# First head of an attention kernel: its loads on three queues, its split in pieces, TensorE turning the identity meanwhile

## The reference

```python
scores = scale * np.matmul(q, k.transpose(0, 1, 3, 2))
thresh = np.max(scores, axis=-1, keepdims=True) - tau
scores = np.where(scores >= thresh, scores, -1000000000.0)
scores = scores - np.max(scores, axis=-1, keepdims=True)
attn = np.exp(scores)
attn = attn / (np.sum(attn, axis=-1, keepdims=True) + 1e-09)
x = np.matmul(attn, v)            # then (tokens, heads * width)
g = gate(x @ w_in);  x = g @ w_out    # twice, with two gates
```

## Time and profile before

| | us |
|---|---|
| median of three runs | 1115.55 (1115.53 to 1116.26) |
| the profiled execution, its own time | 1116.74 |
| its span in the trace | 1115.0 |
| TensorE busy | 1098.8 |
| first matmul starts | 7.68 |

### The profile page before, as it was taken

The page is one execution under the profiler, slowest core; times in us unless marked ns, Lnnn a source line. Parts: engine busy times, 40 slices in busy tenths (PEclk is TensorE's granted clock), DMA queues, the critical chain, the costliest instruction groups (busy, mean ns, idle before and its releaser), DMA issues.

```text
span 1115.0 us, 15233 instructions
## 1 busy us (share of the span) xinstructions
PE 1098.8 (99%) x6064; PEld 880.3 (79%) x6064; DVE 423.6 (38%) x903; ACT 489.9 (44%) x882; POOL 263.5 (24%) x179
## 2 busy tenths in 40 slices
PE   6999999999999999999999999999999999999998
PEld 5767676767668888889988888888888888888897
DVE  6878887878831211112121112123223223222222
ACT  5778787877743332223232234442233233232232
POOL 6686558556621300000000015430000000000000
PEclk9999999999999999999999999999999999999999
DMA  7432223223022000000000022300010010010010
GB/s 221 132 108 65 77 74 97 65 66 96 11 76 76 1 1 1 1 1 1 1 1 1 19 75 96 96 18 1 1 38 1 1 38 0 1 39 1 1 39 20
DMA packets 42488, 46.09 MB, mean 41 GB/s; under 512 B 3504, under 2 KB 30128, under 8 KB 42416
## 3 DMA queue, kind: packets, MB, share of 16 engines
q1 hardware_dynamic: 42416, 45.10, 13.6%
HBM read 40.37 MB, written 4.72 MB: 40 GB/s over the span
## 4 chain that ended last, share of the span: by engine, by line
PE 97%; DVE 1%; ACT 1%; issue 1%; DMA 0%; SPq 0%; DVEq 0%
PE banks L489 35%; PE banks L462 12%; PE banks L464 12%; PE banks L463 12%; PE banks L409 8%; PE banks L356 7%; PE banks L368 5%; PE banks L364 3%; PE banks L389 2%; DVE probs L709 0%; DVE neg_max L725 0%; ACT exps L572 0%; DMA q_raw<-qT 0%; ACT probsT L537 0%; DVE totals L741 0%
## 5 line engine op out<-in xcount | busy, mean ns | idle before, releaser
L770 DVE SCALAR_TENSOR_TENSOR g_low<-gate,g_high 128x512 fp32r<-128x512 f32 (+1 forms) x160 | 102.7, 642 | 473.2 <-ACT g_high L645 473.2
L462 PE MATMUL banks<-x_low,w_in_high 128*128 128x512 f32 (+1 forms) x640 | 235.9, 369 | 0.0
L463 PE MATMUL banks<-x_high,w_in_low 128*128 128x512 f32 (+1 forms) x640 | 235.5, 368 | 0.0
L464 PE MATMUL banks<-x_high,w_in_high 128*128 128x512 f32 (+1 forms) x640 | 235.5, 368 | 0.0
L645 ACT ACTIVATE g_high<-gate 128x512 fp32r<-128x512 f32 (+1 forms) x160 | 94.3, 589 | 309.6 <-PE banks L489 309.1
L462 PEld LDWEIGHTS banks<-x_low,w_in_high 128*128 128x128 f32 x640 | 120.6, 188 | 21.2 <-issue 0.6
L463 PEld LDWEIGHTS banks<-x_high,w_in_low 128*128 128x128 f32 x640 | 120.6, 188 | 20.5
L464 PEld LDWEIGHTS banks<-x_high,w_in_high 128*128 128x128 f32 x640 | 120.7, 189 | 20.0
L725 DVE TENSOR_REDUCE neg_max<-banks 128x1 f32<-128x576 f32 x144 | 108.7, 755 | 50.3 <-PE banks L356 50.1
L489 PE MATMUL banks<-g_low,w_out_high 128*128 128x512 f32 (+1 forms) x320 | 118.0, 369 | 0.8 <-issue 0.8
L489 PE MATMUL banks<-g_high,w_out_low 128*128 128x512 f32 (+1 forms) x320 | 117.8, 368 | 0.0
(11 more groups left out here) (59 smaller groups left out, 1430.1 us busy)
## 6 DMA issues: line engine op xcount, KB each, us to landing
q_raw<-qT SPq DMA_DIRECT2D x64, 144.0 KB, 2.8
k_raw<-kT SPq DMA_DIRECT2D x64, 144.0 KB, 2.8
w_in_raw<-w_in SPq DMA_DIRECT2D x16, 512.0 KB, 4.3
w_out_raw<-w_out SPq DMA_DIRECT2D x16, 512.0 KB, 4.7
out<-x SPq DMA_DIRECT2D x18, 256.0 KB, 2.9
values<-v SPq DMA_DIRECT2D x16, 256.0 KB, 3.1
values<-v SPq DMA_DIRECT2D x16, 32.0 KB, 2.8
tau_in<-tau SPq DMA_DIRECT2D x1, 0.5 KB, 2.8
```

The source lines that it names most:

```text
L462: nc.tensor.matmul(bank, w_in_high[:, t, cols], low, start=(t == 0), stop=False)
L463: nc.tensor.matmul(bank, w_in_low[:, t, cols], high, start=False, stop=False)
L464: mm = nc.tensor.matmul(bank, w_in_high[:, t, cols], high, start=False, stop=(t == KT - 1))
L770: nc.vector.scalar_tensor_tensor(out=g_low[:, f % 2, 0:width], in0=gate[:, f % 2, 0:width], scalar=1 / 6 if layer_of(c) else 1.0, in1=f32( ...
```

## The change

1. **Queues.** k of head 0 is issued by ScalarE as its first two instructions, ahead of its table load; tau is issued by GpSimd ahead of the clearing of `ident`; SP starts with q of head 0.
2. **Split of head 0 in pieces.** ScalarE rounds k in two halves of 288 columns. VectorE's order becomes: q's first 128 columns (scale and round; scale and remainder in one instruction), k's remainder in two halves, and last q's other 448 columns. The in-place scaling of L696 is gone, so the semaphore `q_scaled[0]` gets one increment less, and `split_head` waits for it accordingly. Tile 0 waits for the first q piece and, half by half, for the two k pieces; tile 1 waits for the rest of q.
3. **Turning the identity.** Ahead of tile 0 TensorE does 14 transposes of `ident` against itself into a bank that nobody reads.

```diff
+    WARM = 14
@@ sync
-            sp.dma_start(tau_in[:, :], tau.partition_broadcast(P)).then_inc(tau_loaded, 16)
...
+                if (it, k) == (0, 0):
+
+                    return
                 after(sp, k_low_ready[(k - 2) % HEADS_IT], it + k // 2)
@@ tensor, score_tile
-                if i in (0, MAIN):
+                if t == 0:
+                    pe.wait_ge(first_q_low, 1)
+                if t == 1:
+                    pe.wait_ge(q_low_ready[0], 1)
+                if t > 0 and i in (0, MAIN):
...
+                    if t == 0:
+                        pe.wait_ge((first_k_low, k_low_ready[0])[half], 1)
...
+            for j in range(WARM):
+                nc.tensor.transpose(turned[:, 0:P], ident[:, :], ident[:, :])
@@ scalar
+            for half in range(2):
+                act.dma_start(k_raw[0][DH * half:DH * half + DH, :],
+                              kT[bass.ds(0, 1)].rearrange("a d n -> (a d) n")).then_inc(k_loaded[0], 16)
...
-            round_k(0, 0)
+            act.wait_ge(k_loaded[0], 32)
+            for half in range(2):
+                cols = slice(HALF * half, HALF * half + HALF)
+                nc.scalar.copy(k_high[0][:, cols], k_raw[0][:, cols]).then_inc((first_k_high, k_high_ready[0])[half], 1)
@@ vector
-            q_place = q_stack[0][:, 0:SEQ]
-            nc.vector.tensor_scalar(q_place, q_raw[0][:, :], q_scale[:, :], None, ALU.mult).then_inc(q_high_ready[0], 1)
...
+            def split_first_q(cols, rounded, count):
+
+                place, low = q_stack[0][:, cols], slice(DH, P)
+                nc.vector.tensor_scalar(place, q_raw[0][:, cols], q_scale[:, :], None, ALU.mult).then_inc(rounded, 1)
+                dve.wait_ge(rounded, count)
+                return nc.vector.scalar_tensor_tensor(out=place[low, :], in0=q_raw[0][low, cols], scalar=q_scale[low, :],
+                                                      in1=f32(place[low, :]), op0=ALU.mult, op1=ALU.subtract)
...
+            split_first_q(slice(0, P), first_q_high, 1).then_inc(first_q_low, 1)
+            split_first_k(0, first_k_high).then_inc(first_k_low, 1)
+            split_first_k(1, k_high_ready[0]).then_inc(k_low_ready[0], 1)
+            split_first_q(slice(P, SEQ), q_high_ready[0], 1).then_inc(q_low_ready[0], 1)
@@ gpsimd
+            pool.dma_start(tau_in[:, :], tau.partition_broadcast(P)).then_inc(tau_loaded, 16)
             nc.gpsimd.memset(ident[:, :], 0.0).then_inc(ident_clear, 1)
...
-                pool.wait_ge(q_scaled[k], it + 1)
+
+                pool.wait_ge(q_scaled[k], it + (k > 0))
```

More of the change, by code:

```diff
@@ L158, in attention_and_layers @@
         cleared = sem("cleared")
+        first_k_high = sem("first_k_high")
+        first_k_low = sem("first_k_low")
+        first_q_high = sem("first_q_high")
+        first_q_low = sem("first_q_low")
         ident_clear = sem("ident_clear")
@@ L692, in _, with split_first_k @@
             dve.wait_ge(q_loaded[0], 32)
-            q_place = q_stack[0][:, 0:SEQ]
-            nc.vector.tensor_scalar(q_place, q_raw[0][:, :], q_scale[:, :], None, ALU.mult).then_inc(q_high_ready[0], 1)
[L695 to L700, removed]
+            def split_first_q(cols, rounded, count):
[4 more added lines that the diff above has]
+                                                      in1=f32(place[low, :]), op0=ALU.mult, op1=ALU.subtract)
+            def split_first_k(half, rounded):
+                cols = slice(HALF * half, HALF * half + HALF)
+                dve.wait_ge(rounded, 1)
+                return nc.vector.tensor_tensor(k_low[0][:, cols], k_raw[0][:, cols], f32(k_high[0][:, cols]), ALU.subtract)
+            split_first_q(slice(0, P), first_q_high, 1).then_inc(first_q_low, 1)
+            split_first_k(0, first_k_high).then_inc(first_k_low, 1)
+            split_first_k(1, k_high_ready[0]).then_inc(k_low_ready[0], 1)
+            split_first_q(slice(P, SEQ), q_high_ready[0], 1).then_inc(q_low_ready[0], 1)
             def weigh(t, s):
```

## The result

| | before | changed |
|---|---|---|
| median, same chips | 1116.14 | 1118.91 |
| lowest to highest of 8 | 1115.53 to 1119.45 | 1118.22 to 1120.12 |
| profiled execution | 1116.74 | 1118.22 |
| its span | 1115.0 | 1116.4 |
| first weighing (L709, now L741) starts | 10.65 | 12.15 |

The change made the kernel **slower**: the ratio is 1.0023, 95% interval 1.0013 to 1.0034, some 2.8 us by the medians. The profiled executions are 1.5 us apart; the changed kernel's was the fastest of its eight, and the other's was 0.6 above its median, so the traces show less of the loss than the medians do.

The account below looks back on a forecast made before the run. TensorE was taken as the bound, with only its late start and idle time winnable. A 0.85 us earlier first weighing, nothing given back, took the median from 1115.55 to 1114.7; range 1112.9 to 1115.9.

Parts of the forecast that it names:

- Part 2, the pieces: Split of head 0 on VectorE and ScalarE: TensorE starts at 6.4, tile 1 at 7.9; 0.85 us gain passed on.
- landing L: Common landing of head 0's q and k, taken as 5.2: TensorE starts at L+1.18, q's split ends at L+2.54.
- Part 1, the landing: Loads on separate queues: head 0's q and k both land at 5.2, q 0.3 later, k 0.85 earlier.
- The formula itself: Loads issued at 0.73: B megabytes at rate r land at 0.73 + 2.46 + B/r; undisturbed, 4.42.
- the 249 GB/s of the slow end: DMA rate at the slow limit for two queues, at which head 0's q and k both land at 5.55.
- the second queue moves nothing more: Rival on head 0's loads: q and k both land at 5.55, gain 0.5, 1115.05 us; chance 0.13.
- Head 1: Head 1's q lands at 6.15, 1.35 us earlier, so GpSimd's split of it ends at 12.7, not 14.08.
- the rival with the early clock: Transposes and tiles 0 to 2 raise TensorE's clock early: 2.15 us gain, 1113.4 us; chance 0.27.
- What is late next: After TensorE's first matmul, tile 1 waits for the rest of q until 7.9: 0.85 us gained, not 1.3.
- Part 3, the transposes: 14 transposes before tile 0 take 3.0 us while TensorE is idle: no cost, no earlier clock rise.
- Slower, tau late: Rival: tau on GpSimd's queue, expected 3.5 to 4.7, delays the scale; slower from 5.6, 1118.0 at 8 us; chance 0.06.
- The cap at tile 18: Tile 18 needs head 4, split by 42.19 and taken at 43.00: 0.8 us slack limits gains from an earlier clock.

Follow-up runs that it names:

- GpSimd held: Changed kernel with GpSimd waiting for the end of VectorE's split of head 0 before head 1; 1118.18 us, 2.0 above the kernel before.
- the two light versions: Kernel before with tau on ScalarE's queue, q split whole, k in halves: 1115.95 us; the same plus 24 transposes and ScalarE scaling head 1's q: 1115.04.
- the second execution: Changed kernel, nothing altered, profiled once more: 1119.01 us, span 1117.2.
- 26 transposes: Changed kernel with 26 transposes of the identity instead of 14; 1118.95 us, 2.4 above the kernel before.
- the light version: Kernel before with tau on ScalarE's queue, q split whole in two instructions, k in halves, no transposes; 1115.95 us, ratio 0.9995.
- 28 transposes: Kernel before with 28 transposes of the identity ahead of tile 0 and nothing else; 1116.34 us, 0.2 below before.
- tau moved: Kernel before with only tau's load moved from SP's to GpSimd's queue; median 1116.98 us, ratio 1.0005; its traced execution took 1119.09.

## Why the prediction was wrong

The forecast was 0.85 us faster, the range ended at 1115.9, and the measured median is 1118.9. By its steps:

- **Part 2, the pieces: the step that failed.** It priced q's last 448 columns at 0.44 and 0.62 us, from rows of VectorE taken while GpSimd was idle. In part 1 it had moved GpSimd's start from 7.5 to 6.15, so that GpSimd's first instructions covered the stretch in which VectorE was to do them (6.7 to 7.75), and it never laid the two side by side. Measured: 1.34 and 1.45, **1.73 us more**; held off, 0.45 and 0.68. The chain that it built from a landing L is otherwise right. With GpSimd held and q at 6.19, L+2.54 gives 8.73, and VectorE ended at 8.80.
- **Part 1, the landing: mis-sized.** 5.2 was taken, with 5.55 as the upper end. Measured were 5.78 in the first trace and 5.71 to 6.38 in six others with k on a second queue, against 4.52 to 4.88 with all on SP (tau first on SP, or on ScalarE), and 5.20 with tau alone on GpSimd's queue. The formula itself was good for one queue: 4.42 forecast for q without tau ahead, 4.52 and 4.58 measured. For two queues the 249 GB/s of the slow end was not a lower bound: from 3 to 4 us DMA moved 153 GB/s in the first trace. That tau on GpSimd's queue would delay q was put at nothing, without a row. Cost: 0.6 us in the first trace, and 0.5 to 1.2 in the others. The rival "the second queue moves nothing more" was nearer, and even it was short: with two queues q alone took up to 6.38, where SP alone had both q and k in by 5.82 and 5.95 (the two light versions).
- **Head 1, mis-sized and lost.** Its split was to end at 12.7. It ended at 14.04: its q landed at 6.85 and not at 6.15, and GpSimd lost 0.6 us beside VectorE. At the low clock this cost nothing, since tile 4's scores started only at 16.03, but the rival with the early clock rested on it.
- **Sum.** 0.85 forecast, less 0.58 for the landing, less 1.73 for the collision, is -1.46; the trace shows -1.50. With the commoner landing it is about 2, as in the second execution. The median's 2.8 has 0.5 to 0.8 more that isn't settled. The executions differ in the clock and in the landing of head 4's q (33.8 to 37.5 in fourteen traces), and both can cost over 1 us. With 26 transposes the time goes with the recorded clock, but of the changed kernel's eight executions only the slowest (1120.12, 0.995) has a recorded mean below 1.000, so no run here ties the rest to either.
- **What is late next.** That tile 1 and not tile 0 would be the place was right.
- **Part 3, the transposes.** No earlier rise and no cost: so it was in the first trace, and the median agrees with the kernel without them within its interval. The reason didn't hold: in the second execution the clock was up at tile 0 behind the same 14 transposes, and in the light version it was up at 10.86, behind tiles 0 to 2 and a pause of 0.62 us, the sequence that had not raised it in the kernel before. What kept the gain away was the 2.21 us wait for VectorE, behind which the clock fell. That no earlier rise was seen in the first trace was in part luck.
- **Slower, tau late.** The sign had this mechanism and it was the wrong one: tau landed at 4.75 to 5.0 in the traces of this change instead of 3.56, beyond the 4.7 at the end of its range, and stayed hidden only because q was late too. Another mechanism, not named, gave the sign.
- **The cap at tile 18** stood in a rival and was seen twice: it ate the whole 1.3 us of the 28 transposes, and in one execution with tau moved TensorE waited there for 2.1 us.

## What to carry to other kernels

When a change makes a load land earlier, look up what its arrival starts, and lay that beside what runs then: here VectorE's and GpSimd's splits, which all read SBUF, held each other up when they met (only the 0.13 us of the light version cost nothing), and a row's duration holds only with the neighbour it had. And a second queue, or another engine's queue for a small load, isn't free for the load on the path. An order that looks loose may be tight: VectorE was done 0.02 us after GpSimd began. And a start that is won has to pass every later wait that hangs on another resource; here head 4, fed behind 4 MB of weights, has 0.8 us of slack.

## What the runs showed of the hardware

- Which engine waits depends on who begins. VectorE behind GpSimd took 1.33 to 1.59 us for 0.45 to 0.76; begun 0.1 to 0.4 us ahead of GpSimd it took its full speed (0.45, 0.76), and GpSimd's 1.15 became 1.34 and 1.36. VectorE's maxima and weighings, which read the banks, keep their length beside GpSimd: 0.76 and 0.81 in the kernel before at 9 to 11 us, with GpSimd at work, and 0.75 and 0.81 at 25 to 26 us, with GpSimd idle.
- Two loads of 0.295 MB, started at once on SP's and ScalarE's queues, landed at 5.4 to 6.4 us; the same two in a row on SP's landed at 4.5 to 4.6 and 5.8 to 5.95. With tau on ScalarE's queue in both, taking them apart cost the first 1.1 us and brought the later one nothing (6.21).
- A DMA of 512 bytes issued by GpSimd occupied it for 0.70 us and landed 3.3 to 3.8 us after its start, against 2.8 on SP. In every trace with it DMA moved only 113 to 153 GB/s from 3 to 4 us, against 249 to 307 without, and on an otherwise equal list of loads q landed 0.6 to 0.7 us later.
- TensorE's clock fell from 2.4 to 1.2 GHz behind waits of 1.57 to 2.22 us next to shorter ones, and stayed up behind one of 1.39 us (28 transposes). Dense transposes of the identity raise it as matmuls do. The same 14 transposes, from 2.74 on, raised it in one execution of the changed kernel and not in the other.
- The granted clock column reads 1.00 ahead of the first change that the trace holds, also where matmuls of 288 columns stand 0.24 us apart; only from there on can it be used (0.55 and 0.50 in the second execution of the changed kernel).
